# Attention score rows cut into three equal blocks of 384 keys, in a fused attention, routed-expert and SwiGLU kernel

## The reference, cut to what matters

```python
q_pool = q.reshape(B, H, S // 2, 2, D).mean(axis=3)          # 576 queries a head
scores = scale * np.matmul(q_pool, k.transpose(0, 1, 3, 2))  # 576 x 1152
scores = scores - np.max(scores, axis=-1, keepdims=True)
attn = np.exp(scores)
attn = attn / (np.sum(attn, axis=-1, keepdims=True) + 1e-09)
out = np.matmul(attn, v)
```

## Time and profile before

| | us |
|---|---|
| median of 3 runs | 1481.05 |
| lowest, highest | 1473.97, 1483.73 |
| profiled execution: its time | 1479.3 |
| profiled execution: span, first to last instruction | 1477.5 |
| mean granted TensorE clock, as a share of full speed | 0.967 |

### The profile page before, as it was taken

How to read it: one execution, slowest core, us unless ns; L and a number is a source line. 1 busy time by engine, 2 the same in 40 slices (tenths; PEclk the granted TensorE clock), 3 DMA queues, 4 the chain that set the end, 5 groups by cost and what they waited for, 6 DMA issues and landing times. The chain is left out here.

```text
span 1477.5 us, 24895 instructions
## 1 busy us (share of the span) xinstructions
PE 1383.1 (94%) x7733; PEld 1201.5 (81%) x7734; DVE 873.0 (59%) x1658; ACT 638.0 (43%) x1549; POOL 345.4 (23%) x241
## 2 busy tenths in 40 slices
PE   3999999999999999738988999998999999999998
PEld 2788888888888888626866887887999999999997
DVE  2899999999999998573442444445632323223232
ACT  2788888888888887432034102004421111111111
POOL 3121222222221120278179305022101010100000
PEclk7899999999999999868998999999999999999999
DMA  7566665666666754256257413114510000000000
GB/s 163 124 139 138 138 138 138 146 146 145 146 148 145 195 131 153 101 183 243 86 195 231 128 43 114 43 57 134 146 43 15 29 15 12 28 2 21 0 22 22
DMA packets 128074, 156.85 MB, mean 106 GB/s; under 512 B 47648, under 2 KB 86816, under 8 KB 125984
## 3 DMA queue, kind: packets, MB, share of 16 engines
q1 hardware_dynamic: 112112, 114.35, 30.8%
q10 hardware_dynamic: 12880, 31.99, 6.6%
q0 software_dynamic: 3040, 9.96, 2.1%
HBM read 87.33 MB, written 29.10 MB: 79 GB/s over the span
## 5 line engine op out<-in xcount | busy, mean ns | idle before, releaser
L517 ACT ACTIVATE p_hi<-ps_t 128x512 fp32r<-128x512 f32 (+1 forms) x336 | 194.5, 587 | 69.0 <-PE ps_t L697 65.0
L660 DVE TENSOR_TENSOR p_lo<-ps_t,p_hi 128x512 fp32r<-128x512 f32 (+1 forms) x336 | 216.7, 666 | 11.8 <-ACT p_hi L517 7.9
L581 DVE TENSOR_REDUCE maxima<-ps_s 128x1 f32<-128x512 f32 x288 | 193.6, 685 | 41.4 <-PE ps_s L795 37.6
L541 ACT ACTIVATE probs<-ps_s,neg_max 128x512 f32<-128x512 f32 x288 | 198.7, 690 | 43.4 <-DVE neg_max L594 43.3
L795 PE MATMUL ps_s<-kq_t 128*128 128x512 f32 x640 | 200.0, 414 | 13.4 <-DMA kq_t<-kept_rows 9.4
L697 PE MATMUL ps_t<-ident,probs 128*128 128x128 f32 x1296 | 198.9, 274 | 0.7 <-DVE p_lo L660 0.4
L1030 POOL TENSOR_TENSOR w_parts<-raw_w,w_parts 128x1024 fp32r<-128x1024 f32 x64 | 150.9, 2395 | 186.9 <-ACT w_parts L1100 186.7
L697 PEld LDWEIGHTS ps_t<-ident,probs 128*128 128x128 f32 x1296 | 156.4, 141 | 45.2 <-DVE p_lo L660 9.5
L1646 ACT ACTIVATE silu<-ps_g 128x384 f32<-128x384 f32 x72 | 35.4, 492 | 312.8 <-PE ps_g L1752 312.8
L1699 DVE TENSOR_TENSOR silu<-ps_g,silu 128x384 f32<-128x384 f32 x72 | 40.1, 557 | 210.4 <-ACT silu L1646 210.4
L1100 ACT ACTIVATE w_parts<-raw_w 128x1024 fp32r<-128x1024 f32 x64 | 67.0, 1058 | 219.9 <-PE ps_h L1427 107.1
(11 more groups left out here) (190 smaller groups left out, 2800.3 us busy)
## 6 DMA issues: line engine op xcount, KB each, us to landing
raw_w<-in_moe_w ACTq DMA_DIRECT2D x61, 512.0 KB, 4.1
kq_t<-kept_rows SPq DMA_DIRECT2D x32, 608.0 KB, 6.2
kq_t<-kept_rows SPq DMA_DIRECT2D x32, 320.0 KB, 7.1
raw_k<-in_k SPq DMA_DIRECT2D x32, 288.0 KB, 5.8
raw_v<-in_v SPq DMA_DIRECT2D x16, 576.0 KB, 5.5
kq_t<-kept_rows SPq DMA_DIRECT2D x32, 288.0 KB, 6.4
raw_q<-in_q SPq DMA_DIRECT2D x32, 256.0 KB, 4.1
y_by_slot<-x_out SPq DMA_DIRECT2D x25, 256.0 KB, 2.0
```

The lines of the kernel that those rows point to most:

```text
L517: nc.scalar.activation(p_hi[prob_ring(kind, m)][:, 0:w], T[ring(kind, j)][:, 0:w], ACT.Copy).then_inc(hi_ready, 1)
L541: nc.scalar.activation(probs[:, at:at + 512], S[(2 * tile + h) % SR][:, :], ACT.Exp, bias=neg_max[:, tile:tile + 1], accum_out=sums[par][: ...
L581: nc.vector.reduce_max(maxima[:, 3 * tile + h:3 * tile + h + 1], S[(2 * tile + h) % SR][:, :], AX).then_inc(max_done, 1)
L660: nc.vector.tensor_tensor(p_lo[n][:, 0:w], t[:, 0:w], p_hi[n][:, 0:w].bitcast(F32), ALU.subtract).then_inc(t_free, 1)
```

## The change

The 1152 columns of a tile become three blocks of 384 columns, and `scores_rem`, `exp_rem` and the bank `R` go. The four banks are dealt anew: block 0 of successive tiles takes banks 0 and 3 in turn; block 1 and block 2 have one bank each (1 and 2), which are neighbours, so that VectorE can reduce both in one instruction over 2 x 384 columns. It does so in tiles 1, 2, 4 and 6 (`TOGETHER`); the other five tiles have three single reduces. A tile's exps come in the order block 1, 2, 0 (`EXP_ORDER`). Block b of tile t waits until `3 * (TILES * p + tile - 1) + b` exps are done: block 0 for all those of tile t-2, block 1 for the first exp of tile t-1, block 2 for the second. The wait values of the scores and of the maxima are made the same number, so that a tile's last reduce and its small reduce share one computed value; the body of VectorE's loop of two pairs has 248 instructions. The lists of units, scores, maxima and exps are written anew.

```diff
-    MAIN = 8 * P
+    BLK = SK // 3
...
-        ("g", 0), ("g", 1), ("c", 0), ("c", 1), ("c", 2), ("g", 2), ("a", 0), ("g", 3), ("a", 1),
+        ("g", 0), ("c", 0), ("c", 1), ("g", 1), ("c", 2), ("g", 2), ("g", 3), ("a", 0), ("a", 1),
         ("a", 2), ("x", 0), ("a", 3), ("x", 1), ("a", 4), ("a", 5), ("a", 6), ("a", 7), ("a", 8),
     ]
-    SCORES_AT = [(26, 26), (2, 2), (4, 5), (7, 8), (12, 13), (17, 17), (19, 20), (21, 22), (23, 24)]
-    MAXIMA_AT = [(25, 25), (2, 2), (3, 4), (7, 8), (12, 13), (16, 16), (18, 19), (20, 21), (22, 23)]
-    EXP_AT = [(0, 2, 2), (4, 4, 4), (7, 8, 8), (11, 11, 13), (16, 16, 17), (18, 19, 20), (21, 21, 21), (22, 23, 23), (25, 25, 25)]
+    SCORES_AT = [(25, 26, 26), (2, 2, 2), (5, 5, 5), (6, 8, 8), (9, 10, 11), (12, 14, 15), (16, 18, 19), (21, 22, 22), (24, 24, 24)]
+    MAXIMA_AT = [(24, 25, 25), (2, 2, 2), (4, 4, 4), (6, 7, 7), (10, 11, 11), (13, 13, 14), (18, 18, 18), (21, 21, 21), (23, 23, 23)]
+    TOGETHER = (1, 2, 4, 6)
+    EXP_ORDER = (1, 2, 0)
+    EXP_AT = [(0, 2, 2), (4, 4, 5), (6, 7, 7), (9, 10, 11), (13, 13, 14), (16, 18, 19), (20, 20, 20), (23, 23, 23), (25, 25, 25)]
...
-        S = [ps(f"ps_s{i}", 512) for i in range(SR)]
-        R = ps("ps_r", 512)
+        S_LATE = ps("ps_s_late", 1024)
+        S = [ps("ps_s0", 512), S_LATE[:, 0:512], S_LATE[:, 512:1024], ps("ps_s3", 512)]
...
+        def bank(par, tile, b):
+            return S[b if b else 3 * ((par + tile) % 2)][:, 0:BLK]
...
+                    at = tile * SK + b * BLK
+                    nc.scalar.activation(probs[:, at:at + BLK], bank(par, tile, b), ACT.Exp,
                                          bias=neg_max[:, tile:tile + 1],
+                                         accum_out=sums[par][:, sum_col(tile, b)]).then_inc(exp_done, 1)
...
+                def largest(p, par, tile, b):
+
+                    n = MAXIMA * p + MAXIMUM[tile, b]
+                    if b == 2 and not isinstance(p, int):
+                        n = dve.snap(n)
+                    dve.wait_ge(s_ready, n)
+                    if b == 2 and tile in TOGETHER:
                         nc.vector.tensor_reduce(
+                            maxima[:, 3 * tile + 1:3 * tile + 3],
+                            S_LATE[:, :].rearrange("p (b c) -> p b c", b=2)[:, :, 0:BLK], AX, ALU.max
+                        ).then_inc(max_done, 1)
+                    else:
+                        nc.vector.reduce_max(maxima[:, 3 * tile + b:3 * tile + b + 1], bank(par, tile, b), AX
+                                             ).then_inc(max_done, 1)
+                    if b == 2:
+                        dve.wait_ge(max_done, n)
+                        nc.vector.tensor_reduce(neg_max[:, tile:tile + 1], maxima[:, 3 * tile:3 * tile + 3], AX,
+                                                ALU.max, negate=True).then_inc(bias_ready, 1)
...
+                def scores(p, par, tile, b, opening=False):
+                    if not (opening and (tile == 0 or (tile == 1 and b == 0))):
+                        pe.wait_ge(exp_done, 3 * (TILES * p + tile - 1) + b)
...
+                        at = head * HEAD + b * BLK
+                        last = nc.tensor.matmul(bank(par, tile, b), w, kq_t[par][:, at:at + BLK],
                                                 start=(n == 0), stop=(n == len(ops) - 1))
+                    if (tile, b) in MAXIMUM:
+                        last.then_inc(s_ready, 1)
```

More of the change, by code:

```diff
@@ L104, in attention @@
     TR = 3
-    SR = 3
     LAST = PAIRS - 1
@@ L112, in attention @@
         ("b", 0), ("b", 1), ("b", 2), ("b", 3), ("b", 4), ("b", 5), ("b", 6), ("b", 7), ("b", 8),
[1 row of a table removed]
[1 row of a table added]
         ("a", 2), ("x", 0), ("a", 3), ("x", 1), ("a", 4), ("a", 5), ("a", 6), ("a", 7), ("a", 8),
     ]
-    SCORES_AT = [(26, 26), (2, 2), (4, 5), (7, 8), (12, 13), (17, 17), (19, 20), (21, 22), (23, 24)]
-    MAXIMA_AT = [(25, 25), (2, 2), (3, 4), (7, 8), (12, 13), (16, 16), (18, 19), (20, 21), (22, 23)]
-    EXP_AT = [(0, 2, 2), (4, 4, 4), (7, 8, 8), (11, 11, 13), (16, 16, 17), (18, 19, 20), (21, 21, 21), (22, 23, 23), (25, 25, 25)]
+    SCORES_AT = [(25, 26, 26), (2, 2, 2), (5, 5, 5), (6, 8, 8), (9, 10, 11), (12, 14, 15), (16, 18, 19), (21, 22, 22), (24, 24, 24)]
[3 more added lines that the diff above has]
+    EXP_AT = [(0, 2, 2), (4, 4, 5), (6, 7, 7), (9, 10, 11), (13, 13, 14), (16, 18, 19), (20, 20, 20), (23, 23, 23), (25, 25, 25)]
     assert X_LOADS[X_EARLY - 1][1] * P <= (B - 1) * SQ and (B - 1) * HP <= LAST - 1
     assert w1.shape[2] == PIECE
-    assert HALF_SCALE == 0.25 and len(UNITS) % TR == 0 and 2 * TILES % SR == 0
+    assert HALF_SCALE == 0.25 and len(UNITS) % TR == 0 and 3 * BLK == SK and BLK <= 512
     KEEP = {"first": "ag", "mid": "abcxg", "last": "abcx", "tail": "bcx"}
@@ L164, in lagged @@
         return None if kind == "first" else ("a", CH - LAG + j)
+    taken = [(tile, b) for tile in range(TILES) for b in range(3) if b != 1 or tile not in TOGETHER]
+    MAXIMUM = {at: n + 1 for n, at in enumerate(taken)}
+    MAXIMA = len(taken)
     UNIT_LAST = {"a": ("a", CH - 1), "b": ("b", CH - 1), "c": ("c", 2)}
@@ L222, in attention @@
         s_ready = sem("s_ready")
-        r_ready = sem("r_ready")
         max_done = sem("max_done")
         bias_ready = sem("bias_ready")
-        exp_rem_done = sem("exp_rem_done")
         exp_done = sem("exp_done")
@@ L518, in take, with exps @@
                                          ).then_inc(hi_ready, 1)
[L520 to L530, removed]
+                def exps(p, par, kind, tile, b):
+                    if b == EXP_ORDER[0]:
                         act.wait_ge(bias_ready, TILES * p + tile + 1)
@@ L539, in exp_half @@
                             act.wait_ge(t_filled, upto(p, kind, every, UNIT_LAST["c"]))
-                    at = tile * SK + h * 512
-                    nc.scalar.activation(probs[:, at:at + 512], S[(2 * tile + h) % SR][:, :], ACT.Exp,
+                    at = tile * SK + b * BLK
+                    nc.scalar.activation(probs[:, at:at + BLK], bank(par, tile, b), ACT.Exp,
                                          bias=neg_max[:, tile:tile + 1],
-                                         accum_out=sums[par][:, sum_col(tile, h)]).then_inc(exp_done, 1)
+                                         accum_out=sums[par][:, sum_col(tile, b)]).then_inc(exp_done, 1)
                 def body(p, par, kind):
@@ L551, in body @@
                         for tile in range(TILES):
[L552 to L557, removed]
+                            for at, b in zip(EXP_AT[tile], EXP_ORDER):
+                                if kind != "tail" and at == n:
+                                    exps(p, par, kind, tile, b)
                 for g in range(GROUPS):
@@ L576, in group_lo @@
                     last.then_inc(t_free, 1)
[L578 to L588, removed]
-                        nc.vector.tensor_reduce(
[L590 to L595, removed]
+                def largest(p, par, tile, b):
[4 more added lines that the diff above has]
+                    if b == 2 and tile in TOGETHER:
+                        nc.vector.tensor_reduce(
+                            maxima[:, 3 * tile + 1:3 * tile + 3],
[8 more added lines that the diff above has]
+                                                ALU.max, negate=True).then_inc(bias_ready, 1)
                 def outputs(p, par, kind, unit):
@@ L621, in normalisers @@
                 def normalisers(p, par):
-                    dve.wait_ge(exp_done, 2 * TILES * p)
+                    dve.wait_ge(exp_done, 3 * TILES * p)
                     s3 = sums[1 - par][:, :].rearrange("p (t s) -> p t s", s=3)
@@ L673, in body @@
                                 continue
[L674 to L679, removed]
+                            of = (p, par) if tile else (p + 1, 1 - par)
+                            for b in range(3):
+                                if MAXIMA_AT[tile][b] == n and (tile, b) in MAXIMUM:
+                                    largest(*of, tile, b)
                     if kind == "tail":
@@ L687, in _ @@
                     group_lo(g, g % TR)
-                largest_half(0, 0, 0)
-                largest_half(0, 0, 1)
-                largest_rest(0, 0)
+                for b in range(3):
+                    largest(0, 0, 0, b)
                 over_pairs(dve, body)
@@ L711, in fill @@
                     if what in "ab":
-                        done = 2 * TILES * p + (2 * QT if what == "a" else -2)
+                        done = 3 * (TILES * p + (QT if what == "a" else -1))
                         pe.wait_ge(exp_done, done)
@@ L718, in fill @@
                     elif what == "c":
-                        pe.wait_ge(exp_done, 2 * TILES * p)
+                        pe.wait_ge(exp_done, 3 * TILES * p)
                         last = transposes(t, [probs[:, TC * SK + (3 * i + n) * P:TC * SK + (3 * i + n + 1) * P]
@@ L782, in operands @@
```

(18 more changed lines are left out.)

## The result

The changed kernel takes 1467.86 us (median of 6 runs, 1465.63 to 1470.85), the kernel before 1479.68 (6 runs). The ratio is 0.9919, 95% interval 0.9899 to 0.9939: 0.8% faster, 11.8 us. The interval is 0.2% to either side, so the gain is small but clear of noise. The profiled execution took 1468.12 us with a span of 1466.3, 11.2 less than before.

A forecast was written before the change was run, and what follows sets the result against it. TensorE was taken as the bound, VectorE close behind. A pair of 35.4 us less 0.9 (scores) and 0.2 (net waits) gives 34.3; over 16 pairs 18 us, so the median goes from 1481.05 to 1463, range 1454 to 1480.

The forecast's parts named there:

- TensorE's score work: Attention score matmuls on TensorE: 60 of 384 columns replace 40 of 512 and 20 of 128, 0.9 us less a pair.
- columns alone: Rival, chance 0.07: columns alone set TensorE's price, or 384-column matmuls cost more among transposes; 1478 to 1481 us.
- VectorE's maxima: VectorE's reduces of the score blocks: 23 instructions a pair for 21, same columns, taken as 0.15 us more a pair.
- The turn of the pair: Where one pair passes to the next, TensorE's 0.52 us wait for the copy shrinks: gain 0.3 to 0.5 us.
- the first "a" product: With "g" 3 ahead of "a" 0, the 0.37 us wait before the first product of the "a" units goes.
- New waits: TensorE waits at block 2 of tile 1 and the first "c" product: 0.3 to 1.0 us a pair, 0.7 taken.
- VectorE becomes the bound: Rival, chance 0.25: VectorE, at 33.0 of 34.3 us a pair, takes half of the gain; 1472 us.
- Chained tiles: Rival, chance 0.07: late blocks wait for the previous tile's exps, 0.25 us more in each of nine tiles; 1503 us.
- The wait values: Register and wait work on the sequencers, with 248 instructions in VectorE's loop, was costed at nothing.
- the loop's refetch: Rival, chance 0.03: VectorE's loop fetches its instructions anew at each of 7 turns, 42 us in all; 1505 us.
- Rows 3: Profile rows of VectorE's copy once a pair, 35.34 and 35.46 us apart; read as evidence against a refetch at the loop's turn.
- far row: Profile row of TensorE waiting for instructions, 12.0 us in 2 places, 6 each; used to size a refetch at each turn.

## Why the prediction was right, and where it was off

1463 was predicted, 1468 measured, inside the range of 1454 to 1480; the gain is 12 us of the 18 forecast. The mechanism was the one forecast. The range was drawn wide enough to take in two rivals, and the class that was given the best chance, over 1% faster (0.57), did not come: 0.8% is within 1%, which had 0.34. The forecast's own range of a pair, 33.7 to 34.6 us, was missed by 0.1, and its range in time, 1453 to 1468, just holds the result.

- *TensorE's score work, 0.9 us a pair, "the surest term":* 0.91 by the distances that I used, 0.8 by those over ten pairs. By the first, all versions with 384 columns have 33.24 to 33.31 of work, both old ones with their 512 and 128 columns 34.08 to 34.15; as a count times a distance they could hardly differ more. The distance of 384-column matmuls is 0.175, not 0.173. The rival "columns alone" is out by the run with half rests; that an uncovered weight load is the reason, as the prediction has it, stays open. The result of the formula N/2.4 + 2.5 ns of the Trainium skill ("TensorE: Matmul & The Clock Gate", section "Back-to-back issue gap") is out for these matmuls too: it gives 56 ns where a rest has 106, and 29 where a rest of half the width has 101. That it counts too little at small N is its own caveat.
- *VectorE's maxima, +0.15:* no growth can be read; 550 and 952 ns are as estimated.
- *The turn of the pair, 0.3 to 0.5 gained; the first "a" product, 0.37 gained:* both old waits went, as walked, but the second left 0.16.
- *New waits, 0.3 to 1.0, "I take 0.7":* this is the term that was mis-sized. After the change the waits are 1.46 a pair and not 1.25 or less; "the waits stay near 1.3, 0.2 net" should read 0.1 to 0.2 net the other way. The places that I had named came out larger, or about as named (block 2 of tile 1 0.43 for 0.3, first "c" product 0.31 for 0.4). Missing were block 0 of tile 5 behind the last exp of tile 3 (0.21), tile 0 (0.15) and tile 2 (0.09). My walk took "0.1 in hand" for safe; it had an error of 0.2. The pair is 0.4 us longer than forecast, and 16 x 0.4 = 6 of the 18 us are gone.
- *VectorE becomes the bound:* not so; 3.6 us less of its work bring 0.5, about a third of the waits. But a copy of O that stands behind a subtraction makes its latency count. The time measured lies between this rival's 1472 and the forecast.
- *Chained tiles:* the mechanism is there and small as the lists stand. With the old order of units the kernel is 18 us slower than before, and about half of the marked waits are those that the rival described: from 100 to 560 us TensorE waits 11.0 us for exps ahead of late blocks, and 11.2 for the outputs of "c".
- *The wait values cost nothing, and the loop's refetch, 3 in 100:* right in result, wrong in weight. Rows 3 speak only for a loop of 249 and I had read them as speaking against the mechanism. VectorE's loop of 248 was 10 instructions shorter than one that costs 67 us. The Trainium skill ("Runtime: NRT & Kernel Launch", section "Instruction fetch mechanics") says that instructions come in blocks of 256 and that a branch out of the two loaded blocks stalls; the packets and the idle time of VectorE agree, and so does the count above, if record 64 begins a block, which is inferred from the second gap. It says nothing of what a turn costs; here it is 11.1 us a jump back, more than the 6 of my far row.

## What to carry to other kernels

Equal blocks beat wide ones with a narrow rest where the rest's matmuls cost more than their columns; count the distance between starts, not the row's duration. Where a loop has about 250 instructions or more on an engine, look for gaps behind its jump back after adding an operation: four reduces a pair that by work cost 0.3 us cost 67 us in all. The length alone doesn't tell, as ScalarE's loop of 278 shows; where the loop lies in the engine's list may. A wait in an in-order list can have a second cause just behind the first, so an edit that fails alone may be half of one that works; and an order of units, a layout of banks and the lists that go with them are tried together.

## What the runs showed of the hardware that was not expected

VectorE's loop at 256 instructions cost 3.5 us over 248, at 258 and 266 it cost 67 us: it is a step, not a slope. At each jump back of the slow loops VectorE stands still for 7.5 to 10.0 us, in one piece or in two, TensorE then works for some microseconds at half its clock (0.50 from 219 to 223), and the core loses 11.1. ScalarE's loop of 278 instructions shows no such gap in the same kernels. A reduce over two neighbouring PSUM banks takes 952 ns for 768 columns, the same line as 550 for 384 and 685 for 512.
